# Clustered attention: probability halves of two tiles turned together, and the next pair's q, k and clusters moved to other slots

## Chip, cores and metric

One NeuronCore of a Trainium2 chip. The metric is the device time of one execution in microseconds; lower is better.

## The reference

The program chains three parts: attention masked by clusters, a mixture of experts that sends each token to one expert, and a dense MLP. The change touches the attention alone:

```python
q_assign = np.argmax(np.einsum('bhsd,hcd->bhsc', q_n, c_n), axis=-1)
k_assign = np.argmax(np.einsum('bhsd,hcd->bhsc', k_n, c_n), axis=-1)
mask = q_assign[:, :, :, None] == k_assign[:, :, None, :]
scores = np.where(mask, scale * np.matmul(q, k.transpose(0, 1, 3, 2)), -1000000000.0)
attn = np.exp(scores - np.max(scores, axis=-1, keepdims=True))
attn = attn / (np.sum(attn, axis=-1, keepdims=True) + 1e-09)
return np.matmul(attn, v)
```

Sizes: batch 2, 8 heads, 768 positions, head dimension 64, 16 clusters, all float32.

## The kernel before, in words

**Pairs, tiles, slots.** The 16 heads of both batches are worked in 8 pairs (`PAIRS`; `PPB` = 4 of one batch), 0 to 7. A pair has `TPP` = 12 tiles of 128 queries, six to a head. Every engine runs a loop `body(i)` over the pairs and in it a loop over 12 slots `s`; the order of the instructions in the slots is written out by hand, and each engine executes its own list strictly in order, held back by semaphores only. Three tiles make a group (`GT` = 3, `NG` = 4 groups a pair).

**What a tile passes through.** TensorE computes `scores` two tiles ahead: two matmuls of the q and k stacks (`qa`, `ka`, line 743) and two more (`qb`, `kb`, line 747) that carry the low half of k and the one-hot rows of the clusters, which mask by a large negative term. VectorE takes the row maximum (`maxima`, 1334). ScalarE takes the exponential with the sum of each row (`exps`, 1057). TensorE turns the probabilities in six 128x128 transposes (697), three to PSUM bank 4 (half 0) and three to bank 5 (half 1) (`probs_t`). ScalarE copies each half out as the high part (`probs_high`, 1086) and VectorE subtracts it for the low part (`probs_low`, 1375). TensorE multiplies the turned group by the values, a third of a group a slot, into bank 6 (`values`, 770). ScalarE copies bank 6 out (`out_of_psum`, 1066) and TensorE turns it back by token in bank 7 (`by_token`, fold matmuls, 758), together with the sums for the expert gates; VectorE divides it by the row sums (`normalised`, 1349 and 1352), whose reciprocal is `inverted`, from the sum that GpSimd prepares (`sums`); GpSimd adds the gate's part (`add_logits`).

**Waits of the turning.** A half may be turned when VectorE is done with the same bank of the tile before (`lo_done`), and the first half of a tile when its exponential is done (`p_ready`). In a slot TensorE does: first half of the tile, scores two tiles ahead, second half, extra work, values.

**The next pair.** While pair i runs, pair n = i + 1 is prepared in the same slots: q and k are turned in bank 7 (`transposed`, four parts), copied out by ScalarE (`out_32`), rounded by VectorE (`high`, 1306), the rest computed by GpSimd (`low`, 559). Then SP issues 12 transfers that build the stacks (`stack`, 399). Cluster scores are computed in three parts into bank 7 (`clusters`, 723); VectorE finds their maxima (`cluster_maxima`), GpSimd weights them (`value_clusters`), VectorE picks the first maximum as a one-hot (`pick_clusters`, 1325 and 1330), TensorE turns it (`masks`, 733), ScalarE copies it out (`mask_out`, 1053) and SP stores four more transfers behind the 12 (402, 403). Bank 7 serves all of these and `by_token`, one after the other; ranks of the experts are computed there too, in pair 4. Scores of the next pair begin in slot 10.

**After the attention.** In pair 7 GpSimd also splits the first expert's weights in high and low (`split_piece`, 612 and 616), as soon as SP's transfers of them land. Then follow the expert tiles and the MLP, which the change doesn't touch.

## Time and profile before

| | |
|---|---|
| three runs | 807.22, 807.75, 811.66 us |
| median | 807.75 us |
| profiled execution, its own time | 811.05 us |
| its span in the trace | 809.6 us |
| TensorE matmuls busy | 750.1 us, 93% of the span |
| VectorE, ScalarE, GpSimd busy | 425.4, 371.3, 164.5 us |
| attention, from the first turned probability | 28.55 us to about 295 us |
| a steady pair (pair 3) | 127.69 to 161.02 us |

The profile is of one execution. In a timeline row stand the start, the duration, the engine, the line, the operation, output and inputs, and how many were merged; in brackets how long the engine idled before it and which instruction's end it waited for. The end of a matmul is modelled, about 0.34 us behind the start for 384 columns, so two matmuls that follow each other without a gap overlap in these rows, and the time lost between them is read from start to start. In a row of a stretch stand its length and then the busy time of TensorE's matmuls, its weight loads, VectorE, ScalarE and GpSimd, each with its count, the granted TensorE clock, the busy share of the DMA engines and GB/s.

### The profile page before, as it was taken

Reading aid. Unit: us, or ns where it says so; the run is one execution under the profiler, and the core shown is the slowest. Engines: PE = TensorE matmul, PEld = TensorE weight load, DVE = VectorE, ACT = ScalarE, POOL = GpSimd, SP = SyncE. Lnnn points to the kernel's source line nnn. Section 1 sums busy time; section 2 is a strip of 40 time slices with the busy share of each in tenths; the row PEclk is TensorE's granted clock in tenths of the full one; section 3 lists DMA queues with packets and bytes.
Section 4 is the critical chain, followed back from the end, with each engine's and each line's share of the span. In section 5 each row is a group of like instructions: output and inputs, shape, how many; then the busy total and the mean of one; then the engine's idle time right before and its main releaser. Section 6 shows DMA issues by size and latency. Waiting matters only on the chain.

```text
span 809.6 us, 11950 instructions
## 1 busy us (share of the span) xinstructions
PE 750.1 (93%) x4099; PEld 640.2 (79%) x4099; DVE 425.4 (53%) x791; ACT 371.3 (46%) x707; POOL 164.5 (20%) x253
## 2 busy tenths in 40 slices
PE   4799999999999997679999999999999999999994
PEld 3699899988988875468777878878888888888883
DVE  4587888879878866246464646454322212221221
ACT  2577777777776854256565656463201110110110
POOL 5232242222625874101010101010000100020001
PEclk9999999999999999879999999999999999999998
DMA  8672552835526534864655465160000100010001
GB/s 178 149 173 67 133 124 64 185 70 132 138 68 138 211 116 120 248 236 140 238 179 188 136 217 209 39 208 2 1 0 7 46 0 1 1 53 0 1 1 52
DMA packets 61331, 86.36 MB, mean 107 GB/s; under 512 B 32577, under 2 KB 34769, under 8 KB 60753
## 3 DMA queue, kind: packets, MB, share of 16 engines
q1 hardware_dynamic: 55728, 75.23, 32.9%
q0 software_dynamic: 3376, 6.35, 2.2%
q10 hardware_dynamic: 2160, 3.93, 1.8%
q8 instruction: 38, 0.62, 0.3%
q14 instruction: 29, 0.23, 0.1%
HBM read 56.01 MB, written 9.05 MB: 80 GB/s over the span
## 4 chain that ended last, share of the span: by engine, by line
PE 70%; ACT 6%; DVE 6%; issue 4%; DMA 4%; SPq 4%; POOL 3%; ACTq 2%; another core or an unknown queue 0%; DVEq 0%; POOLq 0%
PE ps L982 16%; PE ps L697 8%; PE ps L997 5%; PE ps L998 5%; PE ps L999 5%; PE ps L770 4%; PE ps L912 4%; PE ps L914 3%; PE ps L913 3%; SPq L399 3%; PE ps L899 2%; PE ps L747 2%; PE ps L901 2%; PE ps L900 2%; PE ps L743 2%
## 5 line engine op out<-in xcount | busy, mean ns | idle before, releaser
L1375 DVE TENSOR_TENSOR pt_l<-ps,pt_h 128x384 fp32r<-128x384 f32 x192 | 105.9, 552 | 41.7 <-ACT pt_h L1086 40.5
L1244 ACT ACTIVATE g<-ps 128x512 f32<-128x512 f32 x48 | 28.7, 598 | 205.4 <-PE ps L982 205.4
L1628 DVE CAST gt_h<-g 128x512 fp32r<-128x512 f32 x48 | 20.5, 427 | 179.7 <-ACT g L1244 179.7
L1086 ACT CAST pt_h<-ps 128x384 fp32r<-128x384 f32 x192 | 92.6, 483 | 43.9 <-PE ps L697 43.8
L697 PE MATMUL ps<-ident,probs 128*128 128x128 f32 x576 | 97.3, 278 | 3.5 <-DVE pt_l L1375 1.9
L1334 DVE TENSOR_REDUCE nmax<-ps 128x1 f32<-128x768 f32 x96 | 91.0, 948 | 7.6 <-PE ps L747 7.6
L1057 ACT ACTIVATE probs<-ps,nmax 128x768 f32<-128x768 f32 x96 | 87.6, 913 | 4.8 <-DVE nmax L1334 4.8
L697 PEld LDWEIGHTS ps<-ident,probs 128*128 128x128 f32 x576 | 70.7, 144 | 17.6 <-DVE pt_l L1375 4.3
L982 PE MATMUL ps<-x2t_h,wl 128*128 128x512 f32 x192 | 74.9, 390 | 0.3 <-DVE wl L1545 0.3
L997 PE MATMUL ps<-wh,gt_l 128*128 128x512 f32 x192 | 74.8, 390 | 0.0
L982 PE MATMUL ps<-x2t_h,wh 128*128 128x512 f32 x192 | 74.7, 389 | 0.0
L999 PE MATMUL ps<-wh,gt_h 128*128 128x512 f32 x192 | 74.7, 389 | 0.0
L982 PE MATMUL ps<-x2t_l,wh 128*128 128x512 f32 x192 | 74.7, 389 | 0.0
L998 PE MATMUL ps<-wl,gt_h 128*128 128x512 f32 x192 | 74.7, 389 | 0.0
L770 PE MATMUL ps<-pt_h,vs 128*128 128x384 f32 x192 | 72.7, 379 | 0.0
L899 PE MATMUL ps<-wh,ht_l 128*128 128x512 f32 x128 | 54.9, 429 | 11.2 <-DVE ht_l L1497 6.1
L770 PE MATMUL ps<-pt_l,vs 128*128 128x384 f32 x192 | 64.7, 337 | 0.0
L912 PE MATMUL ps<-wh,xt_l 128*128 128x512 f32 x128 | 53.3, 416 | 7.0 <-DVE xt_l L1491 6.6
L743 PE MATMUL ps<-ka,qa 128*128 128x384 f32 x192 | 58.1, 384 | 1.2 <-DMA kb<-lo_t 1.2
L1545 DVE TENSOR_TENSOR wl<-raw,wh 128x1024 fp32r<-128x1024 f32 x36 | 42.6, 1221 | 25.6 <-ACT wh L1155 25.6
L1540 DVE TENSOR_TENSOR wl<-raw,wh 128x1024 fp32r<-128x1024 f32 x36 | 42.6, 1220 | 24.3 <-ACT wh L1150 24.1
L747 PE MATMUL ps<-kb,qb 80*128 80x384 f32 x192 | 50.8, 346 | 3.0 <-DMA kb<-onehot_t 3.0
(198 smaller groups left out, 1451.6 us busy)
## 6 DMA issues: line engine op xcount, KB each, us to landing
raw<-in_moe_w SPq DMA_DIRECT2D x32, 1024.0 KB, 7.9
ka<-hi_t SPq DMA_DIRECT2D x32, 192.0 KB
raw<-in_moe_w_in SPq DMA_DIRECT2D x4, 1024.0 KB, 5.8
raw<-in_moe_w_out SPq DMA_DIRECT2D x4, 1024.0 KB, 6.7
xg<-xs ACTq DMA_DIRECT2D x15, 256.0 KB
qn<-in_q SPq DMA_DIRECT2D x16, 192.0 KB, 3.6
kn<-in_k SPq DMA_DIRECT2D x16, 192.0 KB, 3.9
vn<-in_v SPq DMA_DIRECT2D x8, 384.0 KB, 5.0
```

The lines of the kernel that those rows point to most:

```text
L697: return nc.tensor.transpose(dst, src, ident[0:src.shape[0], :] if src.shape[0] < P else ident[:, :])
L743: nc.tensor.matmul(ps[:, bank + half, 0:GQ], qa[par][h][:, rows], ka[par][h][:, half * GQ:(half + 1) * GQ], start=True, stop=False)
L770: last = nc.tensor.matmul(ps[:, 6, 0:GQ], vs[par][:, h * T + c, :], src[gp][:, c, :], start=(c == 0 and src is pt_h), stop=(c == T - 1 and ...
L912: nc.tensor.matmul(ps[:, half, :], xt_l[:, c, :], wh[slot][:, w], start=(c == 0), stop=False)
L982: last = nc.tensor.matmul(ps[:, f % 2, :], a[c // 2][:, w], b[:, c, cols], start=first, stop=(c == DC - 1 and a is wh and b is x2t_h))
L997: nc.tensor.matmul(ps[:, 4 + j, :], gt_l[f % 2][:, tok], wh[slot][:, w], start=(f == 0), stop=False)
L998: nc.tensor.matmul(ps[:, 4 + j, :], gt_h[f % 2][:, tok], wl[slot][:, w], start=False, stop=False)
L999: last = nc.tensor.matmul(ps[:, 4 + j, :], gt_h[f % 2][:, tok], wh[slot][:, w], start=False, stop=(f == FC2 - 1))
L1057: nc.scalar.activation(probs[s % 2][:, :].rearrange("p (a n) -> p a n", a=2), halves(score_bank(s)), ACT.Exp, bias=nmax[:, s % 4:s % 4 + 1 ...
L1086: nc.scalar.copy(pt_h[g % 2][:, half * GT:(half + 1) * GT, t3 * P:(t3 + 1) * P], ps[:, 4 + half, 0:GQ].rearrange("p (c n) -> p c n", c=GT) ...
L1334: nc.vector.reduce_max(nmax[:, s % 4:s % 4 + 1], halves(score_bank(s)), AX.XY, negate=True).then_inc(m_ready, 1)
L1375: nc.vector.tensor_tensor(pt_l[g % 2][at_p], ps[:, 4 + half, 0:GQ].rearrange("p (c n) -> p c n", c=GT), pt_h[g % 2][at_p].bitcast(F32), AL ...
```

## The change

In every slot TensorE turns the second half of the tile before and then the first half of this tile, six transposes in a row, and then the scores; ScalarE and VectorE take the halves in the same order, and the last half 1 is taken after the loops. The value matmuls' parts wait each for the half that they need. q and k of a pair are turned in slots 10 and 11 of the pair two before it and slots 0 and 1 of the pair before it (for pair 1: ahead of the first tile and in slots 0 to 2). Clusters are scored in slots 3 (two parts) and 4 (one) instead of 4 and 5; the one-hot is picked in slot 6 instead of 7 (pair 0: clusters in 4 and 5, pick in 7). The last group of the pair before is turned by token, divided and added in slot 5 instead of 3. VectorE divides ahead of the maximum of its slot. The choice of experts goes from slots 4 and 5 to 6 and 7 of pair 4, and its exponentials from slot 6 to 8.

```diff
-                n = i + 1
+                n, first = i + 1, i == 0
                 for s in range(TPP):
                     g = NG * i + s // GT
+                    if n < PAIRS and s - first in range(4):
+                        low(n, s - first)
                     if s == 0 and i:
                         add_logits(g - 2)
-                    if s == 3 and i:
+                    if s == 5 and i:
                         add_logits(g - 2)
                     if s == 8 or s == 10:
                         add_logits(NG * i + (s - 8) // 2)
                     if s % GT == 1 and g:
                         sums(g - 1)
                     if n < PAIRS:
-                        if s == 1:
-                            low(n, 0)
-                        if s == 2:
-                            low(n, 1)
-                            low(n, 2)
-                        if s == 3:
-                            low(n, 3)
-                        if s == 5:
+                        if s == 4 + first:
                             value_clusters(n)
                         if s == 7:
                             pool.wait_ge(oh_ready, n + 1)
...
 
             def values(g, gp, h, par, part, pair, first_group=False):
 
+                if part < 2:
+                    pe.wait_ge(lo_done, 2 * GT * (g + 1) - 1 + part)
                 if part == 0:
-                    pe.wait_ge(lo_done, 2 * GT * (g + 1))
                     pe.wait_ge(v_done, 2 * pair + 2)
                     if not first_group:
                         pe.wait_ge(ot_done, g)
...
             scores(1, 1, 0)
+            transposed(1, 0, (t_done, 1))
...
+            def probs_t(tile, half):
+
+                if tile:
+                    pe.wait_ge(lo_done, 2 * tile - 1 + half)
+                if half == 0:
+                    pe.wait_ge(p_ready, tile + 1)
+                for c in range(GT):
+                    at_c = half * GT + c
+                    done = tr(ps[:, 4 + half, c * P:(c + 1) * P], probs[tile % 2][:, at_c * P:(at_c + 1) * P])
+                done.then_inc(pt_ready, 1)
...
                 for s in range(TPP):
                     tile = TPP * i + s
-                    pe.wait_ge(p_ready, tile + 1)
-                    probs_t(tile, s, 0)
+                    if tile:
+                        probs_t(tile - 1, 1)
+                    probs_t(tile, 0)
                     if s < TPP - 2:
                         scores(tile + 2, s + 2, par, stacks=i // 2 if s == T - 2 else None)
                     elif not last:
                         scores(tile + 2, s + 2 - TPP, 1 - par, stacks=n // 2 if s == TPP - 2 else None)
-                    if s in (4, 5) and not last:
-                        clusters(n, 2 * (s - 4), ((x32_done, 8) if first else (xn_done, NG * i)) if s == 4 else None)
-                    probs_t(tile, s, 1)
                     if s == 0 and not first:
-                        by_token(NG * i - 2, (xn_done, NG * i - 2))
-                    if not last:
-                        if s == 1:
-                            transposed(n, 1, (x32_done, 4 * n + 1))
-                        if s == 2:
-                            transposed(n, 3, (x32_done, 4 * n + 3))
-                    if s == 3 and not first:
-                        by_token(NG * i - 1, (xn_done, NG * i - 1) if last else (x32_done, 4 * n + 4))
+                        by_token(NG * i - 2, (xn_done, NG * i - 2) if last else (x32_done, 4 * n + 2))
+                    if s == 3 + first and not last:
+                        clusters(n, 0, None)
+                        clusters(n, 1, None)
+                    if s == 4 + first and not last:
+                        clusters(n, 2, None)
+                    if s == 5 and not first:
+                        by_token(NG * i - 1, (xn_done, NG * i - 1) if last else (c_read, n + 1))
                     if s == 8:
                         by_token(NG * i, (xn_done, NG * i) if last else (t_done, n + 1))
+                    if s == 9 and i == PPB:
+                        pe.wait_ge(xn_done, NG * i + 1)
+                        ranks(0)
                     if s == 10:
                         if i == PPB:
                             pe.wait_ge(g_row, 1)
                         by_token(NG * i + 1, (xn_done, NG * i + 1))
-                    if s == 9 and i == PPB:
-                        pe.wait_ge(xn_done, NG * i + 1)
-                        ranks(0)
                     g = s // GT - 1
                     if g >= 0:
                         values(NG * i + g, g % 2, head_of(g), par, s % GT, i, first and g == 0)
                     elif not first:
                         values(NG * i - 1, 1, 1, 1 - par, s % GT, i - 1)
-                    if not last:
-                        if s == 0:
-                            transposed(n, 0, None if first else (xn_done, NG * i - 1))
-                        if s == 1:
-                            transposed(n, 2, (x32_done, 4 * n + 2))
-                        if s == 4:
-                            clusters(n, 1, None)
+                    if first and s < 3:
+                        transposed(1, s + 1, (x32_done, 4 + s + 1))
+                    elif s < 2 and not last:
+                        transposed(n, s + 2, (x32_done, 4 * n + 3) if s else (xn_done, NG * i - 1))
+                    elif s >= TPP - 2 and n + 1 < PAIRS:
+                        transposed(n + 1, s + 2 - TPP, (xn_done, NG * i + 2) if s == TPP - 2 else (x32_done, 4 * n + 5))
                     if s == 7 and not last:
...
@@ -862,6 +858,7 @@
             for i in range(PAIRS):
                 body(i)
             lastg = PAIRS * NG - 1
+            probs_t(PAIRS * TPP - 1, 1)
             by_token(lastg - 1, (xn_done, lastg - 1))
 
             def tile_transpose(t, bank=6):
@@ -871,10 +868,11 @@
                     last = tr(ps[:, bank, c * P:(c + 1) * P], xg[:, c * P:(c + 1) * P])
                 last.then_inc(xt_ready, 1)
 
+            values(lastg, 1, 1, 1, 0, PAIRS - 1)
             pe.wait_ge(lo_done, 2 * PAIRS * TPP)
             tile_transpose(0, bank=5)
-            for part in range(GT):
-                values(lastg, 1, 1, 1, part, PAIRS - 1)
+            values(lastg, 1, 1, 1, 1, PAIRS - 1)
+            values(lastg, 1, 1, 1, 2, PAIRS - 1)
             pe.wait_ge(xtl_done, 1)
             ranks(1)
             by_token(lastg, (xn_done, lastg))
...
+                    g = NG * i + s // GT
+
+                    if s % GT == 0 and g >= 2:
+                        out_of_psum(g - 2, g % 2, None if g < 4 else g - 3)
+                    if first and s < 4:
+                        out_32(1, s, False)
+                    elif s < 3 and not first and not last:
+                        out_32(n, s + 1, False)
+                    elif s == TPP - 1 and n + 1 < PAIRS:
+                        out_32(n + 1, 0, False)
+                    if tile:
+                        probs_high(tile - 1, 1)
+                    probs_high(tile, 0)
                     if s < TPP - 1:
                         exps(tile + 1, s + 1, par)
                     elif not last:
                         exps(tile + 1, 0, 1 - par)
-                    if not last and s == 1:
-                        out_32(n, 1, False)
-                    if not last and s == 2:
-                        out_32(n, 3, False)
-                    probs_high(1)
-                    if not last and s == 0:
-                        out_32(n, 0, False)
-                    if not last and s == 1:
-                        out_32(n, 2, False)
...
-                    if i == PPB and s == 6:
+                    if i == PPB and s == 8:
...
+                    if tile:
+                        probs_low(tile - 1, 1)
+                    probs_low(tile, 0)
+                    if s == 6 + first and not last:
                         pick_clusters(n)
+                    if s in (0, 5) and not first:
+                        normalised(NG * i - 2 + s // 5)
+                    if s in (8, 10):
+                        normalised(NG * i + (s - 8) // 2)
                     if s < TPP - 2:
                         maxima(tile + 2, s + 2)
                     elif not last:
                         maxima(tile + 2, s + 2 - TPP)
-                    done = None
-                    if s in (0, 3) and not first:
-                        done = NG * i - 2 + s // 3
-                        normalised(done)
-                    if s in (8, 10):
-                        done = NG * i + (s - 8) // 2
-                        normalised(done)
-                    probs_low(1)
                     if s == 2 and not first:
                         inverted(NG * i - 1)
                     if s in (7, 9, 11):
                         inverted(NG * i + (s - 7) // 2)
-                    if not last and s == 1:
-                        high(n, 0)
-                    if not last and s == 2:
-                        high(n, 1)
-                        high(n, 2)
-                    if not last and s == 3:
-                        high(n, 3)
+                    if first and s < 4:
+                        high(1, s)
+                    elif s < 3 and not first and not last:
+                        high(n, s + 1)
+                    elif s == TPP - 1 and n + 1 < PAIRS:
+                        high(n + 1, 0)
                     if i == PPB:
-                        if s in (4, 5):
-                            choose(0, s - 4)
+                        if s in (6, 7):
+                            choose(0, s - 6)
```

TensorE, slot 7 of a pair in the middle, up to its second value matmul (`ident,probs` are the turned probabilities, `ka`/`kb` scores, `pt_h`/`pt_l` values); before:

```order
L697 MATMUL ps<-ident,probs 128x128 x3
L743 MATMUL ps<-ka,qa 128x384 x2
L747 MATMUL ps<-kb,qb 128x384 x2
L697 MATMUL ps<-ident,probs 128x128 x3
L770 MATMUL ps<-pt_h,vs 128x384
L770 MATMUL ps<-pt_l,vs 128x384
```

and now:

```order
L692 MATMUL ps<-ident,probs 128x128 x6
L738 MATMUL ps<-ka,qa 128x384 x2
L742 MATMUL ps<-kb,qb 128x384 x2
L766 MATMUL ps<-pt_h,vs 128x384
L766 MATMUL ps<-pt_l,vs 128x384
```

The second three now belong to the tile of this slot, the first three to the tile before.

VectorE, from the low half after the first maxima of the clusters on, through the pick (`nmax` is the row maximum of a tile, `pt_l` a low half); before, slots 6 and 7:

```order
L1334 TENSOR_REDUCE nmax<-ps 128x1
L1375 TENSOR_TENSOR pt_l<-ps,pt_h 128x3x128
L1320 TENSOR_REDUCE cmax<-cval 128x24
L1375 TENSOR_TENSOR pt_l<-ps,pt_h 128x3x128
L1325 TENSOR_TENSOR onehot<-cval,cmax 128x384
L1330 TENSOR_SCALAR onehot<-onehot 128x6x32
L1334 TENSOR_REDUCE nmax<-ps 128x1
L1375 TENSOR_TENSOR pt_l<-ps,pt_h 128x3x128
```

and now, slots 5 and 6:

```order
L1365 TENSOR_TENSOR pt_l<-ps,pt_h 128x3x128 x2
L1345 TENSOR_TENSOR lpart<-ps,rden 128x48
L1348 TENSOR_TENSOR xn<-ps,rden 128x3x64
L1330 TENSOR_REDUCE nmax<-ps 128x1
L1316 TENSOR_REDUCE cmax<-cval 128x24
L1365 TENSOR_TENSOR pt_l<-ps,pt_h 128x3x128 x2
L1321 TENSOR_TENSOR onehot<-cval,cmax 128x384
L1326 TENSOR_SCALAR onehot<-onehot 128x6x32
L1330 TENSOR_REDUCE nmax<-ps 128x1
```

The pick stands behind both low halves, a slot earlier, and still ahead of a maximum; the division (`lpart`, `xn`) stands ahead of its slot's maximum.

TensorE, end of slot 0 and slot 1 of a pair in the middle, up to the next q or k part (`qn`, `kn`: q and k being turned); before:

```order
L697 MATMUL ps<-ident,qn 128x128 x3
L697 MATMUL ps<-ident,probs 128x128 x3
L743 MATMUL ps<-ka,qa 128x384 x2
L747 MATMUL ps<-kb,qb 128x384 x2
L697 MATMUL ps<-ident,probs 128x128 x3
L697 MATMUL ps<-ident,qn 128x128 x3
L770 MATMUL ps<-pt_h,vs 128x384
L770 MATMUL ps<-pt_l,vs 128x384
```

and now, end of slot 10 and slot 11:

```order
L692 MATMUL ps<-ident,qn 128x128 x3
L692 MATMUL ps<-ident,probs 128x128 x6
L738 MATMUL ps<-ka,qa 128x384 x2
L742 MATMUL ps<-kb,qb 128x384 x2
L766 MATMUL ps<-pt_h,vs 128x384
L766 MATMUL ps<-pt_l,vs 128x384
```

q's first part has moved two slots up, and each part has a slot's end of its own.

## Rows read from the trace of the kernel before

**Rows 1.** Pairs 0, 3, 4, 5: us, busy PE, PEld, DVE, ACT, POOL, clock, DMA.
```profile
28.55:60.99 32.44, 31.00 (x210) 28.45 (x211) 26.23 (x51) 24.03 (x55) 9.17 (x14) 1.00 0.72 165
127.69:161.02 33.33, 32.75 (x235) 30.40 (x235) 27.69 (x58) 24.84 (x58) 9.88 (x17) 1.00 0.49 113
161.02:195.46 34.44, 33.12 (x249) 30.88 (x249) 29.42 (x73) 25.10 (x60) 9.89 (x17) 1.00 0.48 111
195.46:231.57 36.11, 33.05 (x236) 30.35 (x236) 29.39 (x66) 24.96 (x58) 16.25 (x23) 1.00 0.43 116
```

**Rows 2.** Timeline, TensorE: slot 11 of pair 3 (start us, us, engine, line, work).
```profile
158.94 0.49 PE L697 MATMUL ps<-ident,probs 128*128 128x128 f32 x3
159.19 0.59 PE L743 MATMUL ps<-ka,qa 128*128 128x384 f32 x2
...
159.98 0.49 PE L697 MATMUL ps<-ident,probs 128*128 128x128 f32 x3
160.23 0.42 PE L770 MATMUL ps<-pt_h,vs 128*128 128x384 f32 x1
...
161.02 0.49 PE L697 MATMUL ps<-ident,probs 128*128 128x128 f32 x3
```

**Rows 3.** Timeline, TensorE and VectorE: end of slot 7, pair 3.
```profile
150.17 0.34 PE L770 MATMUL ps<-pt_l,vs 128*128 128x384 f32 x1
150.93 0.49 PE L733 MATMUL ps<-ident_b,onehot 128*64 128x128 bf16 x6 [0.42 <-issue]
...
150.03 0.55 DVE L1325 TENSOR_TENSOR onehot<-cval,cmax 128x384 bf16<-128x384 f32 x1
150.62 0.21 DVE L1330 TENSOR_SCALAR onehot<-onehot 128x192 bf16<-128x192 bf16 x1
```

**Rows 4.** Timeline, TensorE and VectorE: slots 0 and 1 of pair 4.
```profile
162.39 0.79 PE L758 MATMUL ps<-fold,o_t 128*128 128x80 f32 x6
...
163.59 0.33 PE L770 MATMUL ps<-pt_l,vs 128*128 128x384 f32 x1
164.06 0.52 PE L697 MATMUL ps<-ident,qn 128*128 128x128 f32 x3
...
166.63 0.34 PE L770 MATMUL ps<-pt_l,vs 128*128 128x384 f32 x1
166.95 0.30 PE L697 MATMUL ps<-ident,kn 128*128 128x128 f32 x1
...
163.45 0.20 DVE L1349 TENSOR_TENSOR lpart<-ps,rden 128x48 f32<-128x48 f32 x1
163.57 0.35 DVE L1352 TENSOR_TENSOR xn<-ps,rden 128x192 f32<-128x192 f32 x1
```

**Rows 5.** Timeline, TensorE and SP's queue: slot 10 of pair 5 ([idle before <-releaser]).
```profile
227.32 0.62 PE L747 MATMUL ps<-kb,qb 80*128 80x384 f32 x2 [1.59 <-DMA kb<-onehot_t]
...
221.75 1.42 SPq L399 DMA_DIRECT2D kb<-lo_t  x1
```

**Rows 6.** Timeline, TensorE: slot 6 of pair 4, slot 0 of pair 5.
```profile
182.07 0.30 PE L697 MATMUL ps<-ident,probs 128*128 128x128 f32 x1 [0.73 <-DVE pt_l L1375]
...
199.21 0.52 PE L697 MATMUL ps<-ident,qn 128*128 128x128 f32 x3 [0.83 <-DVE xn L1352]
```

**Rows 7.** Timeline, ScalarE: slot 11 of pair 3.
```profile
159.47 0.48 ACT L1086 CAST pt_h<-ps 128x384 fp32r<-128x384 f32 x1 [0.99 <-PE ps L697]
159.84 0.91 ACT L1057 ACTIVATE probs<-ps,nmax 128x768 f32<-128x768 f32 x1
160.64 0.20 ACT L1057 ACTIVATION_READ_ACCUMULATOR probs<-ps,nmax 128x1 f32 x1
```

**Rows 8.** Timeline, GpSimd: pair 7.
```profile
266.95 1.04 POOL L612 CAST wh<-raw 128x1024 fp32r<-128x1024 f32 x1 [1.95 <-DMA raw<-in_moe_w]
...
295.98 0.53 POOL L580 TENSOR_SCALAR rden<-rsum 128x3 f32<-128x3 f32 x2
```

**Rows 9.** Stretch within the expert tiles, columns as in group 1.
```profile
338.90:345.60 6.70, 5.65 (x14) 4.43 (x15) 3.05 (x3) 2.69 (x5) 1.14 (x2) 0.50 0.61 247
```

56 lines of the change are left out of this document (22 added, 34 removed).

## The prediction

> **What bounds the kernel now.** Read the stretches of the pairs first. The reader is to see that in the attention part TensorE is busy for 32.75 us of the 33.33 us of a pair, with VectorE at 27.69 and ScalarE at 24.84, and the clock granted at 1.00 [rows 1]. "Busy" hides small losses, because a matmul's end is modelled about 0.34 us after its start; the start-to-start distances of the timeline show them. A slot without extra work takes 161.02 - 158.94 = 2.08 us [rows 2]: three transposes, four score matmuls, three transposes, four value matmuls. None of it is idle, so such a slot has nothing to give. Six transposes cost the same whether they stand together or in threes: the scores begin 0.25 us after the first of three, and the distance from 159.19 to 159.98 is that of four matmuls of about 0.18 each plus the rest of the last transpose. Grouping as such is therefore booked at nothing.
>
> What can be had is the time in which TensorE stands still. In a steady pair three places have a price:
> - **The masks.** The last value matmul starts at 150.17, the first mask transpose at 150.93: 0.76 where a turn is 0.18, so 0.58 lost. VectorE finished the one-hot at 150.62 + 0.21 = 150.83 [rows 3]. It was asked for in the same slot.
> - **The q transposes in slot 0.** 163.59 to 164.06 is 0.47, so 0.29 lost; they wait for the normalisation, which began at 163.57 and took 0.35 [rows 4].
> - **The k transposes in slot 1.** 166.63 to 166.95 is 0.32, so 0.14 lost, waiting for ScalarE to empty bank 7 [rows 4].
>
> Single places are dearer. Pair 4 takes 34.44 us and pair 5 takes 36.11 [rows 1]: in pair 5 the one-hot rows of the keys arrive late and TensorE idles 1.59 us, and the last of the transfers that stand before them on SP is issued until 221.75 + 1.42 = 223.17, some 1.7 us before TensorE's slot begins [rows 5]. TensorE also idles 0.73 us in slot 6 of pair 4, for VectorE's low half, and 0.83 us in slot 0 of pair 5, for the normalisation [rows 6]. Pair 0 takes 32.44 us [rows 1] although it has no value matmuls in slots 0 to 2 (three times 0.79, rows as in a plain slot, 160.23 to 161.02 [rows 2], so 2.4 us less work than pair 3): it loses at least 1.5 us more than pair 3 does.
>
> **The change, part by part.** TensorE's instructions are the same in number and kind; only their order moves, so the sum is made of waits.
>
> 1. *One-hot a slot earlier.* Clusters go to slots 3 and 4, the pick on VectorE to slot 6, the masks stay in slot 7. Between pick and masks there is now more than a slot, so of 0.58 I leave 0.05: gain 0.53 in each of pairs 1 to 6. In pair 0 the clusters come a slot later and the pick stays in slot 7, now behind both low halves: no gain there.
> 2. *q and k turned from slot 10 on.* The transposes of slot 0 and 1 now wait for ScalarE's copy of the slot before, which ScalarE does first in its slot: 0.14 goes. The wait for the normalisation occurs twice, in slots 10 and 0, but VectorE now normalises ahead of its maximum. Today the maximum delays it: the six fold matmuls end at 162.39 + 0.79 = 163.18, the normalisation begins at 163.45 [rows 4]. Begun at 163.2 it would end 0.2 to 0.25 sooner. So 0.29 becomes about 0.10, twice: net gain 0.09. Together 0.23 a pair.
> 3. *Order on ScalarE.* Now the second half of the tile before and the first half of this one are both copied ahead of the exponential. The ring is: first transpose of a tile's first half to the copy 159.47 - 158.94 = 0.53, copy to exponential 0.37, exponential to the end of its accumulator read 160.64 + 0.20 - 159.84 = 1.00, to the next tile's transposes about 0.1 [rows 2, 7]: 2.0 us against a slot of 2.08. In the new order the earlier half comes in 0.33 us ahead, its copy takes a turn of 0.37, so the copy that counts slips by only 0.04 to 0.05, and the ring still closes at 2.05 to 2.08. Where a copy of bank 6 or 7 stands ahead of both (slots 2, 6 and 9 have such a copy and no extra work on TensorE) I book 0.06 lost, 0.18 a pair. Slots 0, 1, 10 and 11 have such copies too, but 0.3 us or more of extra TensorE work to hide them.
> 4. *Order on VectorE.* The pick (150.03 to 150.83, 0.7 to 0.8 with the start of what follows [rows 3]) stands ahead of the maximum in slot 6, a slot without extra TensorE work. The maximum of tile 8 comes 0.7 late, its exponential about 0.5 late, where the ring leaves nothing but the 0.4 us of masks in slot 7: 0.1 lost. VectorE has 33.33 - 27.69 = 5.6 us of slack in a pair, so it catches up in slot 8. Half-1 results are needed one slot later than before by the value matmuls, which absorbs the rest. Today's smaller waits behind the cluster maxima (slot 6 after slot 5) go to set against this: I book 0.1 for slots 6 to 8 and gain 0.3 for those, and so nothing net after the 0.18 of point 3.
> 5. *Sum of a steady pair*: 0.53 + 0.23 = 0.76, rounded to 0.8. Pairs 1 to 6: 4.8 us. Ends of it: nothing (each wait moves rather than goes) and 1.4.
> 6. *Pair 0*: 0.2 from point 2, nothing from point 1, and of the 1.5 or more that it loses beyond a steady pair, 1.0: its transposes now stand before the first tile, where TensorE waits for the first exponential, and one at a time after. 1.2, between 0 and 2.0.
> 7. *Pair 4*: the choice of experts moves from slots 4 and 5 to 6 and 7 and leaves the cluster maxima, but meets the pick: of 0.73 I take 0.4, between -0.5 and 0.9.
> 8. *Pair 5*: the low halves of q and k are done a slot sooner, so SP's 12 stack transfers start 2 us or more sooner and end before the mask rows are there. The 1.59 goes, and 0.2 of the 0.83: 1.8, between 0 and 2.3.
> 9. *Pair 7*: nothing. GpSimd splits the first expert's weights from 266.95 on, without a break until its sum at 295.98 [rows 8], and the last sums wait for it. TensorE may run ahead but ends no sooner. What counts is when GpSimd can start, and that is when the weights land after the last mask transfer; SP is free a little earlier: gain 0.4.
> 10. Last group's sums in slot 5 and the tail (one value part ahead of the wait for the last half): hidden behind point 9. Nothing; at most 0.5 either way.
>
> Sum: 4.8 + 1.2 + 0.4 + 1.8 + 0.4 = 8.6 us. The profiled execution took 811.05 us, so it would give 802.5. The median of the three runs shown is 807.75, 3.3 us below, and the MoE stage explains that size of scatter: 6.7 us stretches at half clock follow idle waits there (338.9 to 345.6, clock 0.50 [rows 9]), and each costs up to 6.7 / 2 = 3.4 us. Against the median the forecast is 807.75 - 8.6 = **799.2**.
>
> **The rivals.**
> - *A, half of it.* VectorE is the second busiest engine; the pick ahead of a maximum and both low halves back to back push each wait along. Then the 0.76 a pair falls to about 0.2 and only the single places (pairs 0, 4, 5) pay: 6 x 0.2 + 1.0 + 0.4 + 1.8 = 4.4, time **803.4**. For: 27.69 of 33.33 busy. Against: 5.6 us slack. Chance 0.12.
> - *B, nothing arrives.* The gain waits at GpSimd: if the weights' transfer, not SP's place in the queue, sets 266.95 (POOL idled 1.95 us for it [rows 8]), earlier attention only lengthens that wait. The transfers are issued after the mask rows, so they should move along. **807**. Chance 0.06.
> - *C, ScalarE's ring opens: slower.* The exponential of the next tile stands behind two copies. If the first copy is taken late (its half waits for bank 5 to be free), the second starts not 0.05 but up to 0.37 later, or more with VectorE behind. The ring is then 2.4 or more and every slot with no or little extra work stretches: three plain and two with 0.33 to 0.42 of extra. It decides from 8.6 / (8 x 3) = 0.36 us a plain slot; at 0.6 and 0.25: 8 x (3 x 0.6 + 2 x 0.25) = 18 us lost against 8.6 gained, time **817**. For: the ring is within 0.1 of the slot. Against: bank 5 was freed a slot before. Chance 0.05.
> - *D, the clock falls: slower.* Today six transposes stand in a row (q's three from 164.06, then the tile's three [rows 4]) and the clock stays at 1.00 [rows 1]; the change makes that nine. One stretch at 0.50 a pair as in [rows 9] would cost 7 x 3.4 = 24 against the 8.6: **823**. Chance 0.02. The Trainium skill, "TensorE: Matmul & The Clock Gate", section "Part 4: PE-mode transpose", says that transposes do not count as busy for the clock in the way matmuls do; by that rule a denser run of them speaks against this change. The trace has no fall in any attention pair.
>
> **How the numbers follow.** The forecast's own case has 0.75: 794 to 803. All upper ends together would be 8.4 + 2.0 + 0.9 + 2.3 + 0.4 + 0.5 = 14.5 us, which I don't believe, so 794; the low ends of pairs 0, 4 and 5 leave 4.8 - 0.5 + 0.4 = 4.7, so 803. The range takes in A and the scatter of one half-clock stretch above, and leaves out B's upper side, C and D: 794 to 806. About 0.5% (4 us) is what a measurement of this kernel can tell from no change; the bound is 803.7. Faster: 0.75 less the part lost to a stray half-clock stretch, plus half of A: 0.80. Same: half of A, B and the rest: 0.13. Slower: 0.07.
>
> **What would show it.** Right: masks following the value matmuls within 0.25 us in slot 7; a pair of 32.5 us instead of 33.33; no idle before the score matmuls of pair 5, slot 10; GpSimd's first split at about 258 instead of 266.95 and its last sum 29 us later; all else shifted. Wrong: a plain slot over 2.12 us, with the transposes waiting for the exponential (C); low halves late, with transposes waiting for them in slots 7 to 9 (A); GpSimd's first split still at 266 (B); a granted clock under 1.00 within the attention (D).

## The result, and the profile after

The changed kernel took 802.06 us (median of five runs, 799.89 to 802.94), the kernel before, measured beside it, 809.01 us (five runs, 807.22 to 811.66). The ratio is 0.9908, 95% interval 0.989 to 0.9926, so about 7 us less. Measured together once more, they took 801.96 and 809.17 us, ratio 0.990 (0.9878 to 0.9921). The profiled execution took 799.89 us, its span is 798.4, against 811.05 and 809.6 before; it is the fastest of its five, while 811.05 lies near the slow end of the kernel before.

The stretches of pairs 0, 3, 4, 5, 6 and 7 after the change, columns as in [rows 1]:

```profile
28.48:59.90 31.42, 30.39 (x210) 28.44 (x211) 25.65 (x51) 23.97 (x56) 9.23 (x14) 1.00 0.76 175
125.08:157.68 32.60, 32.60 (x236) 31.11 (x235) 27.68 (x58) 24.89 (x58) 10.03 (x17) 1.00 0.51 116
157.68:191.51 33.83, 33.09 (x249) 31.37 (x248) 30.27 (x73) 25.26 (x60) 10.01 (x17) 1.00 0.49 113
191.51:225.41 33.90, 32.75 (x236) 31.05 (x235) 30.07 (x66) 25.04 (x58) 16.48 (x23) 1.00 0.47 129
225.41:257.23 31.82, 31.82 (x230) 30.52 (x229) 27.46 (x58) 24.22 (x55) 16.63 (x24) 1.00 0.54 136
257.23:284.56 27.33, 27.02 (x185) 25.25 (x183) 23.37 (x48) 23.79 (x55) 26.36 (x22) 1.00 0.43 143
```

A steady pair went from 33.33 to 32.60 us, and by the modelled ends TensorE is now busy for all of it. Pair 0 went from 32.44 to 31.42, pair 4 from 34.44 to 33.83, pair 5 from 36.11 to 33.90. The clock is granted at 1.00 from the first record of it on, and that record begins at 30.18 us here and at 31.66 us before. The column of a stretch shows 1.00 also where there is no record; the distances of the transposes show that the start of pair 0 ran at the lower clock. The kernel before, then the changed one:

```profile
30.50 0.84 PE L697 MATMUL ps<-ident,probs 128*128 128x128 f32 x3
31.13 0.76 PE L697 MATMUL ps<-ident,qn 128*128 128x128 f32 x3
...
30.33 0.49 PE L692 MATMUL ps<-ident,qn 128*128 128x128 f32 x3
30.66 0.82 PE L692 MATMUL ps<-ident,probs 128*128 128x128 f32 x6
```

Three transposes take 0.63 us there and 0.33 here. In another trace of this study, that of the small VectorE operations below, the record covers that stretch and has 0.50:

```profile
27.58:31.02 3.44, 3.44 (x14) 3.34 (x15) 1.89 (x4) 2.15 (x5) 0.00 (x0) 0.50 0.74 170
```

Where it came from, TensorE in slots 7 and 10 of pair 3 and in slot 0 of pair 4 (the counterparts of [rows 3, 4]):

```profile
146.42 0.33 PE L766 MATMUL ps<-pt_l,vs 128*128 128x384 f32 x1
146.69 0.52 PE L728 MATMUL ps<-ident_b,onehot 128*64 128x128 bf16 x6
...
154.66 0.33 PE L766 MATMUL ps<-pt_l,vs 128*128 128x384 f32 x1
154.92 0.52 PE L692 MATMUL ps<-ident,qn 128*128 128x128 f32 x3
...
160.23 0.33 PE L766 MATMUL ps<-pt_l,vs 128*128 128x384 f32 x1
160.49 0.52 PE L692 MATMUL ps<-ident,kn 128*128 128x128 f32 x3
```

The masks follow the last value matmul after 0.27 us, where it was 0.76; the turns in slots 10 and 0 after 0.26, where the q turn of slot 0 took 0.47 and the k turn of slot 1 0.32.

What the change did not bring is in pairs 4 and 5. VectorE, GpSimd and TensorE there:

```profile
178.85 1.05 DVE L1421 TENSOR_TENSOR leq<-logit,lmax 128x48 f32<-128x48 f32 x1
179.94 1.02 DVE L1365 TENSOR_TENSOR pt_l<-ps,pt_h 128x384 fp32r<-128x384 f32 x2
...
192.67 0.95 DVE L1464 TENSOR_SCALAR esum<-esum 128x6 f32<-128x6 f32 x1
...
178.84 1.96 POOL L551 TENSOR_TENSOR vs<-vn,vs 128x384 fp32r<-128x384 f32 x2
...
192.58 1.01 POOL L559 TENSOR_TENSOR lo_t<-x,hi_t 128x384 fp32r<-128x384 f32 x1 [3.54 <-DVE hi_t L1302]
...
180.55 1.01 PE L692 MATMUL ps<-ident,probs 128*128 128x128 f32 x6 [0.74 <-DVE pt_l L1365]
...
195.55 0.52 PE L692 MATMUL ps<-ident,kn 128*128 128x128 f32 x3 [1.15 <-DVE xn L1348]
```

Two operations on 48 and on 6 elements a partition took 1.05 and 0.95 us, and each ended within 0.08 us of a GpSimd subtraction's end (179.90 against 178.84 + half of 1.96 = 179.82; 193.62 against 193.59). TensorE waited 0.74 us behind the first and 1.15 behind the second. The kernel before had the same two at 0.21 and 0.17 us, with GpSimd idle:

```profile
176.07 0.21 DVE L1429 TENSOR_TENSOR leq<-logit,lmax 128x48 f32<-128x48 f32 x1
...
196.70 0.17 DVE L1472 TENSOR_SCALAR esum<-esum 128x6 f32<-128x6 f32 x1
```

The end of the attention part (GpSimd as in [rows 8], then VectorE and TensorE behind pair 7):

```profile
256.87 1.05 POOL L612 CAST wh<-raw 128x1024 fp32r<-128x1024 f32 x1
...
285.94 0.53 POOL L580 TENSOR_SCALAR rden<-rsum 128x3 f32<-128x3 f32 x2
...
286.20 0.18 DVE L1334 RECIPROCAL rden<-rden 128x3 f32<-128x3 f32 x1 [1.23 <-POOL rden L580]
286.30 0.53 DVE L1365 TENSOR_TENSOR pt_l<-ps,pt_h 128x384 fp32r<-128x384 f32 x1
...
286.88 0.66 PE L692 MATMUL ps<-ident,xg 128*128 128x128 f32 x4 [0.20 <-DVE pt_l L1365]
...
291.11 0.48 PE L910 MATMUL ps<-wh,xt_l 128*128 128x512 f32 x1
```

GpSimd's splits begin 10.1 us sooner (266.95 before) and its last sums follow 29.1 us later, as before. Pair 7 itself starts 8.0 us sooner, and the first hidden matmul 8.7 us (299.81 before). The rest of the profiled 11.2 us lies in the expert tiles, and it isn't the change's: from the first hidden matmul to the first matmul of the MLP it is 232.8 us in the trace before and 230.3 after, and between 230.1 and 233.2 in the thirteen traces of this study, in an order that follows no kernel.

### The profile page after: what moved, and what is told of

The parts are those of the page before. It is cut to its first block, busy times and chain, and to the rows that moved or that the text cites. A ratio compares the mean times of both kernels' runs of the same rounds, so it can differ in the third digit from the quotient of the medians.

```text
span 798.4 us, 11944 instructions
## 1 busy us (share of the span) xinstructions
PE 748.6 (94%) x4099; PEld 645.2 (81%) x4099; DVE 426.7 (53%) x791; ACT 371.9 (47%) x707; POOL 165.6 (21%) x253
## 4 chain that ended last, share of the span: by engine, by line
PE 82%; DVE 4%; ACT 3%; issue 3%; DMA 2%; ACTq 2%; POOL 1%; SPq 1%; another core or an unknown queue 0%; DVEq 0%; POOLq 0%
PE ps L980 16%; PE ps L692 11%; PE ps L766 8%; PE ps L995 5%; PE ps L997 5%; PE ps L996 5%; PE ps L742 4%; PE ps L738 4%; PE ps L910 4%; PE ps L912 3%; PE ps L911 3%; PE ps L718 3%; PE ps L897 2%; PE ps L898 2%; PE ps L899 2%
## 5 line engine op out<-in xcount | busy, mean ns | idle before, releaser
L1365 DVE TENSOR_TENSOR pt_l<-ps,pt_h 128x384 fp32r<-128x384 f32 x192 | 97.9, 551 | 32.5 <-ACT pt_h L1078 31.1
L1078 ACT CAST pt_h<-ps 128x384 fp32r<-128x384 f32 x192 | 84.4, 486 | 31.1 <-PE ps L692 30.9
L692 PE MATMUL ps<-ident,probs 128*128 128x128 f32 x576 | 83.2, 276 | 1.6 <-DVE pt_l L1365 0.7
L692 PEld LDWEIGHTS ps<-ident,probs 128*128 128x128 f32 x576 | 66.7, 141 | 9.7 <-DVE pt_l L1365 3.0
L766 PE MATMUL ps<-pt_h,vs 128*128 128x384 f32 x192 | 68.9, 359 | 0.0
L681 POOL DMA_INDIRECT out<-zeros,row_token x3 | 3.0, 995 | 245.1 <-ACT zeros L1250 157.5
```

What stands on the lines that cost most here:

```text
L692: return nc.tensor.transpose(dst, src, ident[0:src.shape[0], :] if src.shape[0] < P else ident[:, :])
L766: last = nc.tensor.matmul(ps[:, 6, 0:GQ], vs[par][:, h * T + c, :], src[gp][:, c, :], start=(c == 0 and src is pt_h), stop=(c == T - 1 and ...
L1078: nc.scalar.copy(pt_h[g % 2][:, half * GT:(half + 1) * GT, t3 * P:(t3 + 1) * P], ps[:, 4 + half, 0:GQ].rearrange("p (c n) -> p c n", c=GT) ...
L1365: nc.vector.tensor_tensor(pt_l[g % 2][at_p], ps[:, 4 + half, 0:GQ].rearrange("p (c n) -> p c n", c=GT), pt_h[g % 2][at_p].bitcast(F32), AL ...
```

## The experiments

### The pick and the normalising put back

```diff
-                    if s == 6 + first and not last:
+                    if s == 7 and not last:
                         pick_clusters(n)
```

> The changed kernel, with the one-hot of the clusters back in slot 7 of every pair (it stands in slot 6 of pairs 1 to 6 now). Theory (step 1 of the prediction): the mask transposes of slot 7 wait for it again. In slot 6 it ended 2.9 us after the slot's start, and the value matmuls of slot 7 end 2.05 us after theirs, so about 0.85 us of wait in each of pairs 1 to 6, nothing in pair 0: 5.1 us, 807 us against 802. Lower bound: the 0.58 of the kernel before, 3.5 us. Rival: the maximum of slot 6 comes 0.65 us earlier without the pick ahead of it, and ScalarE and TensorE use that up, so that less than 0.2 us per pair stays (under 803.5).

Measured: 804.89 us, ratio to the kernel before 0.9959 (0.9946 to 0.9972). In the trace a steady pair takes 0.58 us more than 32.60:

```profile
127.29:160.47 33.18, 32.64 (x236) 31.11 (x235) 27.76 (x58) 24.81 (x58) 10.03 (x17) 1.00 0.50 113
```
```profile
149.50 0.49 PE L728 MATMUL ps<-ident_b,onehot 128*64 128x128 bf16 x6 [0.54 <-issue]
...
149.19 0.21 DVE L1326 TENSOR_SCALAR onehot<-onehot 128x192 bf16<-128x192 bf16 x1
```

The wait came back at the size of the kernel before (3.5 us over six pairs), the lower bound. Without the pick in slot 6 the maximum there comes earlier, and the two low halves of slot 7 begin 1.04 us behind the slot's start instead of 1.60 (147.67 behind 146.63; 146.02 behind 144.42 in the changed kernel); that pays for the second low half that now stands ahead of the pick. Step 1 stands.

```diff
-                    if s in (0, 5) and not first:
-                        normalised(NG * i - 2 + s // 5)
-                    if s in (8, 10):
-                        normalised(NG * i + (s - 8) // 2)
                     if s < TPP - 2:
                         maxima(tile + 2, s + 2)
                     elif not last:
                         maxima(tile + 2, s + 2 - TPP)
+                    if s in (0, 5) and not first:
+                        normalised(NG * i - 2 + s // 5)
+                    if s in (8, 10):
+                        normalised(NG * i + (s - 8) // 2)
```

> The changed kernel, with the normalising of slots 0, 5, 8 and 10 behind the maximum of its slot again. Theory (step 2): the q and k turns of slots 10 and 0 wait for it, 0.19 us longer in each of the two by the prediction's working (1.2 to 2.4 us over six pairs, 803 to 804.5). Rival: in the new order the maximum ends 2.9 us after its slot's start, and the turns stand 2.3 to 2.7 us after theirs, so that the wait grows by 0.6 us in each of slots 0 and 10: 7 to 8 us, 809 to 810. Third: nothing.

Measured: 809.68 us, 1.0027 (1.0009 to 1.0045). The pair, and the two turns in it:

```profile
128.11:162.01 33.90, 32.78 (x236) 31.13 (x235) 27.55 (x58) 24.89 (x58) 10.00 (x17) 1.00 0.49 111
```
```profile
159.27 0.52 PE L692 MATMUL ps<-ident,qn 128*128 128x128 f32 x3 [0.46 <-DVE xn L1348]
...
165.58 0.52 PE L692 MATMUL ps<-ident,kn 128*128 128x128 f32 x3 [0.67 <-DVE xn L1348]
```

1.30 us in a steady pair (0.53 in slot 10, 0.76 in slot 0): the rival was right. From pair 0 to pair 6 this trace is 9.0 us longer than that of the changed kernel, so this one line of order is worth as much as the whole change. The prediction had it at 0.2 a turn, from the position of the maximum in the old order.

### Grouping undone, and grouping alone

Grouping undone in the changed kernel, on TensorE (ScalarE and VectorE alike):

```diff
-                    if tile:
-                        probs_t(tile - 1, 1)
                     probs_t(tile, 0)
                     if s < TPP - 2:
                         scores(tile + 2, s + 2, par, stacks=i // 2 if s == T - 2 else None)
                     elif not last:
                         scores(tile + 2, s + 2 - TPP, 1 - par, stacks=n // 2 if s == TPP - 2 else None)
+                    probs_t(tile, 1)
...
```

> The changed kernel with the grouping alone undone: the second half of a tile's probabilities is turned in its own slot again, behind the scores, on TensorE, ScalarE and VectorE; all else stays. The prediction booked the grouping at nothing, so by it 802 plus or minus 1. Rival: the other moves live on the grouping. The pick and the normalising now stand ahead of the maximum, and with it ahead of the second low half, so that this half comes 0.4 to 0.8 us later in five slots of a pair, and the next slot's second transposes wait for their bank: 0.5 to 1.5 us per pair, 806 to 812.

Measured: 808.14 us, 0.9992 (0.9978 to 1.0006). The pair, and TensorE in its slot 7:

```profile
128.10:162.02 33.92, 32.98 (x236) 30.52 (x235) 27.69 (x58) 24.85 (x58) 9.98 (x17) 1.00 0.49 111
```
```profile
149.62 0.55 PE L692 MATMUL ps<-ident,probs 128*128 128x128 f32 x3 [0.69 <-DVE pt_l L1361]
```

The low half that stands behind maximum, pick or normalising is late for the next slot's second transposes, and TensorE waits 0.35 us in slot 6, 0.8 in slot 7 and 0.35 in slot 9. Without the grouping the rest of the change gives next to nothing.

The reverse, the kernel before with the same three pieces of grouping and nothing else:

> The kernel before with the grouping alone: the second half of a tile is turned, taken over by ScalarE and subtracted by VectorE at the start of the next slot, six transposes in a row; every other step stays in its slot and its order. Prediction: the grouping as such is worth nothing, 0.999 to 1.001 of the kernel before. Rival 1: it carries the gain by itself (the low halves no longer stand behind the maximum, so that the waits of slots 6 and 7 go): 0.3 to 0.8 us per pair, ratio 0.992 to 0.997. Rival 2: half a tile later costs the value matmuls a wait: slower, 1.003 or more. The run without the grouping (808 against 802) says that the other moves need it; this one says whether it needs them.

Measured: 814.77 us, 1.0068 (1.0044 to 1.0091), 5.4 us slower than the kernel before. The pair, then slots 0, 1 and 7:

```profile
128.79:163.09 34.30, 32.66 (x235) 30.98 (x234) 27.57 (x58) 24.79 (x58) 9.98 (x17) 1.00 0.48 109
```
```profile
132.29 0.52 PE L697 MATMUL ps<-ident,qn 128*128 128x128 f32 x3 [0.55 <-DVE xn L1358]
...
135.51 0.52 PE L697 MATMUL ps<-ident,kn 128*128 128x128 f32 x3 [0.32 <-ACT x L1047]
...
152.91 0.49 PE L733 MATMUL ps<-ident_b,onehot 128*64 128x128 bf16 x6 [0.78 <-issue]
```

So the four corners, a steady pair and the ratio of the whole kernel:

| | halves in their own slot | halves grouped |
|---|---|---|
| other steps as before | 33.33 us, 1 | 34.30 us, 1.0068 |
| other steps as changed | 33.92 us, 0.9992 | 32.60 us, 0.9908 |

Each side by itself lengthens a steady pair, by 0.97 and 0.59 us; together they take 0.73 off. Over the whole kernel the moves without the grouping can't be told from no change. Grouping puts two low halves ahead of the maximum on VectorE. What the next slot's transposes wait for is then first in line, but everything behind the maximum comes a half later, and that must be moved ahead of it or a slot earlier. With the halves apart the same moves push the second low half back.

How far one move goes with the grouping, the kernel before with grouping and normalising ahead of the maximum:

> The kernel before with the grouping and with the normalising of slots 0, 3, 8 and 10 ahead of the maximum (ahead of it and of nothing else; q, k, clusters and pick stay where they were). With the grouping alone a pair took 34.32 us against 33.35: TensorE waited 0.82 us in slot 0 (the q turn, for the normalised group), 0.51 in slot 1 (the k turn, for a ScalarE copy), 0.83 in slot 7 (the masks). Theory: the grouping puts two low halves ahead of the maximum, so what stands behind the maximum is late; the normalising ahead of it mends slot 0 (0.82 to about 0.15) and nothing else: a pair of 33.6 to 33.7, ratio to the kernel before 1.001 to 1.004, so that the q and k turns and the pick are what makes the rest of the way to 32.60. Rival: the normalising is all that the grouping needs, 33.1 or less, ratio under 0.998.

Measured: 810.43 us, 1.0012 (0.9997 to 1.0028), and a pair (pair 2; pair 3 took 33.67):

```profile
95.37:129.05 33.68, 32.60 (x235) 31.01 (x234) 27.79 (x58) 24.79 (x58) 9.95 (x17) 1.00 0.49 113
```

The theory was met in the pair; the time excludes the rival, and can't be told from the kernel before. From 33.33 the way is: grouping +0.97, normalising ahead -0.62 (34.30 to 33.68), the pick a slot earlier -0.58 (first experiment), and the remaining 0.50 for the q, k and cluster slots, which is about the 0.51 that TensorE loses in slot 1 for the k turn. The pick's share is taken over from the changed kernel, and the last is a difference: q, k and the clusters were never moved by themselves.

### Router steps and GpSimd

```diff
-                        if s == 7:
+                        if s == (8 if i == PPB else 7):
                             pool.wait_ge(oh_ready, n + 1)
                             split_v(n)
...
+                    if i == PPB and s == 11:
+                        gate(0, 0)
+                    if i == PPB + 1 and s == 0:
+                        gate(0, 1)
                     if first and s < 4:
                         high(1, s)
...
-                        if s == 11:
-                            gate(0, 0)
-                    if i == PPB + 1:
-                        if s == 0:
-                            gate(0, 1)
```

> The changed kernel, with VectorE's small router steps kept apart from GpSimd's long ones: the value split of pair 4 a slot later, and the two gate steps of slots 11 (pair 4) and 0 (pair 5) ahead of the high half that releases GpSimd's low half. Theory: two small VectorE operations took 1.05 and 0.95 us where 0.2 and 0.17 are usual, both while a GpSimd subtraction of 128x384 ran, and TensorE waited for them (0.83 us in slot 7 of pair 4, 1.35 in slot 0 of pair 5); apart, they take 0.2 and 0.17 again, slot 7 loses its 0.8 and slot 0 about 0.75: 1.5 us less, 800.5. Rival: they were long for another reason and stay long wherever they stand (802). Second rival: slot 0 of pair 5 was as long in the kernel before without such a long operation, so only the 0.8 of pair 4 goes (801.2).

Measured: 799.06 us, 0.9889 (0.9872 to 0.9905). The two operations, in the places of 1.05 and 0.95:

```profile
179.08 0.21 DVE L1420 TENSOR_TENSOR leq<-logit,lmax 128x48 f32<-128x48 f32 x1
...
191.79 0.17 DVE L1463 TENSOR_SCALAR esum<-esum 128x6 f32<-128x6 f32 x1
```

Pairs 4 and 5 together went from 67.73 to 66.06 us, 1.67 less: the theory, with both places. The shares are slot 7 of pair 4, 3.54 to 2.72 us, and slot 0 of pair 5, 4.39 to 3.63. It is the trace that shows this; the intervals of the two ratios, 0.9889 here and 0.9908, overlap. This trace then lost 0.86 us in slots 7 and 8 of pair 6, where ScalarE took a finished bank 1.2 us late; why is open (last section).

The mechanism by itself:

```diff
...
                         probs_low(tile - 1, 1)
+                    if s == 7 and not last:
+                        if i in (1, 3):
+                            nc.vector.tensor_tensor(probe[:, i, :], zeros[:, 0:48], zeros[:, 48:96], ALU.mult)
+                        elif i == 5:
+                            nc.vector.tensor_scalar(probe[:, i, :], zeros[:, 0:48], 1.0, None, ALU.add)
+                        else:
+                            nc.vector.reduce_max(probe[:, i, 0:6], zeros[:, 0:48].rearrange("p (a n) -> p a n", a=6), AX.X)
                     probs_low(tile, 0)
```

> The changed kernel with one needless small VectorE operation in slot 7 of pairs 0 to 6, between the two low halves, at a time when GpSimd subtracts 128x384 (a column of results that nobody reads): a product of two 128x48 pieces of SBUF in pairs 1 and 3, a 128x48 scalar addition in pair 5, a 128x48 maximum in pairs 0, 2, 4 and 6. Theory: an operation with two inputs from SBUF, or the scalar addition, can't start while GpSimd works and ends with GpSimd's current operation: 0.5 to 1.7 us instead of 0.2, and TensorE stands 0.4 to 0.9 us in slot 8 of pairs 1, 3 and 5; the maximum takes 0.2 us and costs under 0.15. Rival: all of them take 0.2 us, and the long operations of the router had another cause. Second rival: all kinds are held alike.

Measured once (803.31 us). Pair 3, pair 2, pair 5, each with GpSimd's row of the time:

```profile
146.83 0.82 DVE L1380 TENSOR_TENSOR probe<-zeros 128x48 f32<-128x48 f32 x1
...
146.58 1.96 POOL L552 TENSOR_TENSOR vs<-vn,vs 128x384 fp32r<-128x384 f32 x2
...
114.23 0.19 DVE L1384 TENSOR_REDUCE probe<-zeros 128x6 f32<-128x48 f32 x1
...
113.98 1.97 POOL L552 TENSOR_TENSOR vs<-vn,vs 128x384 fp32r<-128x384 f32 x2
...
215.06 0.25 DVE L1382 TENSOR_SCALAR probe<-zeros 128x48 f32<-128x48 f32 x1
...
214.76 0.96 POOL L548 CAST vs<-vn 128x384 fp32r<-128x384 f32 x2
```

The product of two SBUF operands was held until GpSimd's first subtraction ended (146.58 + 0.98 = 147.56, the product at 147.65); TensorE lost 0.35 us for it in slot 8, just under what was expected. The maximum, in the same place, took 0.19 us and cost nothing in pair 2 (0.11 us in pairs 0 and 4). The scalar addition fell into a GpSimd cast, 0.2 us before that cast's first half ended, and shows nothing either way (slot 8 of that pair was 0.63 us longer, but behind a copy that ScalarE took 0.95 us late); that such an operation is held too rests on the 0.95 us of pair 5 and on its 0.17 once moved. The many low halves of the timeline, which read one operand from PSUM, kept their 0.55 us beside GpSimd's subtractions (147.57 in this trace, and 82.00 in pair 1). The Trainium skill, "SBUF — State Buffer", section "SBUF: two separate sides", has this rule: VectorE and GpSimd share a pair of ports that one instruction holds from start to end, and it concerns VectorE operations in a two-port mode, or with two inputs in SBUF against a GpSimd operation that reads SBUF. Its part "Who interferes with whom" adds that on this chip a reduction never contends. The runs agree, with 0.82 against 0.19 us.

### Two small moves, and all three

The by-token product of slot 10 ahead of the scores:

```diff
+                    if s == 10 and i != PPB:
+                        by_token(NG * i + 1, (xn_done, NG * i + 1))
                     if s < TPP - 2:
                         scores(tile + 2, s + 2, par, stacks=i // 2 if s == T - 2 else None)
...
-                    if s == 10:
-                        if i == PPB:
-                            pe.wait_ge(g_row, 1)
+                    if s == 10 and i == PPB:
+                        pe.wait_ge(g_row, 1)
                         by_token(NG * i + 1, (xn_done, NG * i + 1))
```

> The changed kernel with the by-token product of slot 10 ahead of the slot's scores instead of behind them (not in pair 4). What is left of the wait of slot 10 (0.24 us a pair, the q turn waits for the normalised group) goes, since the product and with it the normalising come 0.7 us earlier: 0.24 x 7 = 1.7 us, 800.4. Rival: the scores come 0.66 us later, the maximum of slot 10 with them, and slots 11 and 0 wait instead: 802 or more.

Measured: 799.85 us, 0.9888 (0.9853 to 0.9923). In the trace slot 10 of a steady pair is 3.19 us instead of 3.28 and its other slots are as they were, so 0.09 a pair, not 0.24. The q turn now follows without a gap:

```profile
153.25 0.34 PE L766 MATMUL ps<-pt_l,vs 128*128 128x384 f32 x1
153.42 0.49 PE L692 MATMUL ps<-ident,qn 128*128 128x128 f32 x3
```

It follows after 0.17 us, where it was 0.26, so its wait was 0.09 and is gone whole. The rest of the 0.24 was never the turn's: it lies in the slot's six probability transposes, whose scores begin 0.70 us behind the first of them in the changed kernel (151.99 to 152.69), against 0.58 in slot 11. The rest of the difference to 802 is scatter within the intervals.

The last x32 copy of a pair behind the exponentials of slot 2:

```diff
-                    elif s < 3 and not first and not last:
+                    elif s < 2 and not first and not last:
                         out_32(n, s + 1, False)
...
+                    if s == 2 and not first and not last:
+                        out_32(n, 3, False)
```

> The changed kernel with ScalarE's last x32 copy of a pair behind the exponentials of slot 2 instead of ahead of its high halves (pairs 1 to 6). Theory: of the 0.3 us that TensorE loses in slot 3, 0.11 is the wait for the exponentials that this copy delays; it goes, 0.11 x 6 = 0.7 us, 801.4. Rival: the clusters of slot 3, which need this copy, wait for it instead, 0.1 to 0.4 us a pair: 802.5 to 804.5.

Measured: 801.14 us, 0.9899 (0.9874 to 0.9925). Slot 3 is 3.92 us instead of 3.98: half of what was expected, which is under what the times can tell: inconclusive by them, right in sign by the trace.

The three together, and the changed kernel once more, measured beside them:

> The changed kernel with the three small moves together: router steps kept apart from GpSimd (fourth run of this study), by-token product first in slot 10 (seventh), last x32 copy behind the exponentials (eighth). By the traces 0.82 + 0.76 us in pairs 4 and 5, 0.09 a pair and 0.06 a pair: 1.6 + 0.6 + 0.4 = 2.6 us below the changed kernel in the same call, ratio of the two 0.996 to 0.9975. Rival: GpSimd's weight splits of pair 7 start with the raw weights' arrival, not with the pair, and take it all back: the two alike.

> The changed kernel as it is, for the comparison on the same chip: 802 (799 to 804), 0.989 to 0.993 of the kernel before.

Measured: 798.00 us (796.63 to 799.37), 0.9853 (0.9835 to 0.987) of the kernel before; the changed kernel 801.96, 0.990 (0.9878 to 0.9921). The three are 4.0 us below the changed kernel, somewhat more than the 2.6 worked out, and the intervals don't touch. A pair of the three (pair 2) takes 32.40:

```profile
93.22:125.62 32.40, 32.40 (x237) 31.17 (x236) 27.68 (x58) 24.79 (x58) 9.99 (x17) 1.00 0.52 117
```

It is the fastest kernel of the study. GpSimd's first split began at 256.20 in its trace and at 258.16 in that of the changed kernel beside it, and the first hidden matmul at 290.42 and 292.39, so the gain reached the end of the attention part, against the rival. That is 2.0 us of the 4.0; where the rest lies is open.

## Why the prediction was right, and where it was wrong

The forecast was 799.2 us with 794 to 806; the time was 802.06. The sum was 8.6 us, and the trace has 8.7 up to the first hidden matmul (299.81 to 291.11). The forecast was set against the median of three runs, 807.75; with more runs the kernel before had medians of 807.7 to 809.4, and where both kernels were measured together the difference is 7.0 and 7.2. So the sum was some 1.5 us too large by the times. The second trace of the changed kernel shows where such an amount can go: its first hidden matmul is at 292.39, only 7.4 sooner, and 1.15 us of it went in slots 7 and 8 of pair 5, behind a copy that ScalarE took late (last section). That the first trace agrees to 0.1 us is luck, as its parts show:

| | booked | in the trace |
|---|---|---|
| pair 0 | 1.2 | 1.02 |
| pairs 1 to 3 | 2.4 | 2.25 |
| pair 4 | 1.2 | 0.61 |
| pair 5 | 2.6 | 2.21 |
| pair 6 | 0.8 | 1.83 |
| pair 7 up to the first hidden matmul | 0.4 | 0.71 |

The rest of the 8.7 is pair 0's start, 0.07 sooner. Pair 6 gave what pairs 4 and 5 fell short of. By the prediction's steps:

1. **One-hot a slot earlier**, 0.53 a pair. Right: slot 7 went from 3.34 to 2.72 us, and undone it costs 0.58; nothing gained in pair 0, as said (the pick stays in slot 7 there, which takes 3.54 us against 3.34 before).
2. **q and k turned from slot 10 on**, net 0.23 a pair. Right as a net (slots 0 and 1 lost 0.36 + 0.17 us of TensorE's time before, slots 10 and 0 lose 0.24 + 0.13 now: 0.16 gained), and mis-sized inside. "Begun at 163.2 it would end 0.2 to 0.25 sooner" priced the normalising by the old order. In the new one both low halves stand ahead of the maximum, so the normalising behind it would be 0.65 late, in two slots: 1.30 us a pair.
3. **Order on ScalarE**, 0.18 a pair lost. Too dark: slots 2, 6 and 9 take 2.06 to 2.07 us, so the ring closes and nothing is lost. What was missed is slot 3 with two parts of the clusters, where TensorE now loses some 0.3 us (3.98 us, against 3.71 for the slot that had two parts before). Of it 0.06 went when the copy of slot 2 was put behind the exponentials; the rest is open.
4. **Order on VectorE**, nothing net. Right in sign: slot 6 is 2.06 instead of 2.23 us. Points 3 and 4 together were booked at nothing; slots 3 to 5 took 9.41 us and take 9.66, so with slot 6 it is 0.08 lost.
5. **Steady pair**, 0.76. Measured 0.73.
6. **Pair 0**, 1.2. Measured 1.02, with one turn of 0.33 us more in it than before, but the mechanism was wrong. The 1.5 us that it lost beyond a steady pair were put down to its waits; TensorE ran at half clock from 28.55 to 31.66, which alone is an estimated 3.11 / 2 = 1.55 us. Now it is 28.48 to 30.18, 0.85 by the same estimate, so 0.70 of the 1.02 is the clock, whose rise varies: in the seven traces with the changed kernel's first pair (slot 10 of it apart) the clock is up between 27.47 and 32.39 us, and pair 0 takes 30.82 to 32.27. About 0.3 is left for the order. **Pair 6**, which the sum counts as a steady pair, went from 33.65 to 31.82; 0.66 of this is that it has two turns less, which the prediction did not book.
7. **Pair 4**, 0.4 for the choice of experts. Failed: 34.44 to 33.83 is 0.61, less than the 0.73 of the plain pair. The wait of slot 6 [rows 6] went, and a wait as long (0.74) came in slot 8. The step feared the pick ahead of the choice; what met it was GpSimd's value split, which the pick releases.
8. **Pair 5**, 1.8. The DMA wait of 1.59 [rows 5] is gone, as said: the last mask transfer of the stacks was issued at 218.76, before TensorE's slot 10 began at 219.72. Of the 0.83 in slot 0 [rows 6] nothing went; it is 1.15 now, for the gate's step held by GpSimd. Measured 2.21 for the pair, against 0.76 + 1.8.
9. **Pair 7**, 0.4: 0.71 from its start to the first hidden matmul (34.59 to 33.88 us). GpSimd's chain moved by 10.1 us, more than the pair. SP came to the weights 9.0 us sooner (259.98 to 250.94), and where GpSimd waited 1.95 us for them before, its first split now follows its indirect DMA at once.
10. **Tail**: nothing in size, but a wait is new. The last low half (286.30) stands behind the reciprocal that waits for GpSimd's sum, and TensorE waits 0.20 us for it; before, that low half was done at 294.5 and nothing waited.

The step that failed as a statement is the first paragraph's "Grouping as such is therefore booked at nothing". It is true for TensorE's own time, six transposes cost what three and three do, and the sum didn't need more. As a claim on the change it was wrong by 5.4 us one way and some 6 us the other: alone it makes the kernel slower, and without it the other moves give nothing. The sum was not hurt, because only the whole change was priced: the cost of the grouping and the gain of the moves meet in it.

Of the rivals, A is refuted by the pair of 32.60, B by GpSimd's start, C by the slots of 2.06 us, D by the clock at 1.00 in every pair of this trace from 30.18 on, though nine transposes now stand in a row (154.92 and 155.27 above are three and six).

## What to carry to other kernels

When an order on one engine changes, price each moved step in the complete new order of its queue, and read an added step's cost on what stands behind it; parts of such a change can each lose or give nothing alone and win together, so undo them one at a time before one is dropped. A small VectorE operation with both inputs in SBUF should not be put where GpSimd has just been released to a long one: here it lasted until that one ended, and what stood behind it on VectorE paid.

## What the chip showed that was not expected

- The holding of VectorE by GpSimd, above: 0.82, 0.95 and 1.05 us for operations of 0.17 to 0.21.
- A fall of the clock inside the attention part. In the trace of the first experiment ScalarE took a finished bank 1.9 us late in slot 7 of pair 6. TensorE stood 2.39 us, did nothing but the twelve transposes of masks and probabilities until 254.40, and then had half the clock for 3.4 us:

```profile
253.35 0.49 PE L728 MATMUL ps<-ident_b,onehot 128*64 128x128 bf16 x6 [2.39 <-issue]
```

  The stretch behind it:

```profile
254.40:257.80 3.40, 3.40 (x16) 3.40 (x15) 1.57 (x5) 1.92 (x5) 2.08 (x3) 0.50 0.23 44
```

  The 1.59 us for which TensorE stood in pair 5 of the kernel before [rows 5] had no such sequel; the granted clock stayed at 1.00.
- Late ScalarE copies. In eight of the thirteen traces, nine places, all in slot 7 of pair 5 or 6, ScalarE took a turned half between 0.95 and 2.0 us after TensorE had finished it, though by the program the copy waits for nothing else. TensorE lost 0.45 to 1.3 us for it in slots 7 and 8, and 3.4 in the trace above. All eight are traces of the changed kernel or of variants of it with the grouping; its first trace is the only one of these without such a copy, and the kernel before, its two grouped variants and the ungrouped one have none. GpSimd was issuing indirect DMAs shortly before each, but it does so in the traces without a late copy too. The cause stays open; so does whether it is what the changed kernel's other executions lose against the profiled one (799.89 us against a median of 802.06).
